# Turning r unscaled and multiplying the powers of the decay in where it leaves PSUM

## The reference

```
for t in range(768):
    cur   = (u * k[t]) outer v[t]
    y[t]  = r[t] @ (state + cur)
    state = w * state + k[t] outer v[t]
```

## Time and profile before

| | us |
|---|---|
| median of 3 runs | 996.05 (994.66 to 996.93) |
| profiled execution, first to last instruction (span) | 962.4 |
| median of the runs less that span | 33.65 |
| PE busy, of the span | 905.8 |
| POOL busy, of the span | 341.3 |
| DVE busy, of the span | 416.5 |
| ACT busy, of the span | 255.9 |

### The profile page before, as it was taken

One profiled execution on the slowest core, in us unless ns is written; L12 is line 12 of the kernel. 1 busy time (PEld: TensorE's weight loads), 2 busy tenths in 40 slices (PEclk: granted clock), 3 DMA queues, 4 the chain that ended last, 5 costly groups with the idle time before them and its releaser, 6 DMA issues.

```text
span 962.4 us, 19802 instructions
## 1 busy us (share of the span) xinstructions
PE 905.8 (94%) x6919; PEld 856.9 (89%) x6920; DVE 416.5 (43%) x697; ACT 255.9 (27%) x511; POOL 341.3 (35%) x276
## 2 busy tenths in 40 slices
PE   6899998898998999999979999999999999999998
PEld 6777787697897888988878999999999999999998
DVE  7767766536655547264244222222232223222221
ACT  1333332122222222222233222222222222222222
POOL 6799996577444326065346010010100001000000
PEclk9999999999999999999999999999999999999999
DMA  8885565353324132224221010000100001000000
GB/s 198 224 223 129 129 163 186 85 167 113 133 85 155 39 133 82 82 62 150 93 80 29 22 42 9 25 25 0 49 0 25 25 18 31 0 25 0 25 1 25
DMA packets 115583, 74.20 MB, mean 77 GB/s; under 512 B 79248, under 2 KB 109840, under 8 KB 115552
## 3 DMA queue, kind: packets, MB, share of 16 engines
q1 hardware_dynamic: 101312, 48.01, 18.2%
q10 hardware_dynamic: 10720, 14.95, 4.3%
q0 software_dynamic: 3520, 10.82, 4.0%
HBM read 57.44 MB, written 16.32 MB: 77 GB/s over the span
## 4 chain that ended last, share of the span: by engine, by line
PE 67%; POOL 12%; issue 7%; DVE 6%; DMA 3%; POOLq 2%; DVEq 1%; SPq 1%; ACT 1%; ACTq 0%
PE bank L1187 20%; PE bank L1189 20%; PE bank L1188 20%; POOL w_lo L501 3%; POOL w_lo L552 3%; DMA xs<-x_rows,token_of 2%; POOL k_pad L486 2%; POOL r_pad L488 2%; POOL ruk L491 2%; PE bank L1239 1%; PE bank L1083 1%; POOL xs L531 1%; POOLq L549 1%; SPq L401 1%; DVE w_hi L832 1%
## 5 line engine op out<-in xcount | busy, mean ns | idle before, releaser
L1187 PE MATMUL bank<-bT_hi,f_hi 128*128 (+1 forms) x576 | 194.7, 338 | 0.0
L1188 PE MATMUL bank<-bT_lo,f_hi 128*128 (+1 forms) x576 | 192.8, 335 | 0.0
L1189 PE MATMUL bank<-bT_hi,f_lo 128*128 (+1 forms) x576 | 192.6, 334 | 0.0
L890 DVE TENSOR_TENSOR act<-silu,bank 128x384 f32<-128x384 f32 x96 | 53.2, 554 | 252.1 <-PE bank L1189 252.1
L552 POOL TENSOR_TENSOR w_lo<-raw,w_hi x72 | 99.0, 1408 | 111.1 <-DVE w_hi L832 107.0
L571 POOL DMA_INDIRECT xg<-y_slots,slot_of x24 | 25.0, 1040 | 277.4 <-DVE xg_s L874 256.2
L1188 PEld LDWEIGHTS bank<-bT_lo,f_hi 128*128 128x128 f32 x576 | 108.5, 188 | 0.0
L1187 PEld LDWEIGHTS bank<-bT_hi,f_hi 128*128 128x128 f32 x576 | 108.4, 188 | 0.0
L1189 PEld LDWEIGHTS bank<-bT_hi,f_lo 128*128 128x128 f32 x576 | 108.4, 188 | 0.0
L1187 PE MATMUL bank<-f_hi,act_hi 128*128 128x384 f32 x288 | 96.8, 336 | 2.5 <-DVE act_lo L893 2.5
L1189 PE MATMUL bank<-f_hi,act_lo 128*128 128x384 f32 x288 | 96.7, 336 | 0.0
(11 more groups left out here) (169 smaller groups left out, 1464.6 us busy)
## 6 DMA issues: line engine op xcount, KB each, us to landing
raw<-in_moe_w_dram SPq DMA_DIRECT2D x16, 1536.0 KB, 6.7
y_slots<-y_out ACTq DMA_DIRECT2D x28, 192.0 KB, 1.9
k_in<-in_k_dram SPq DMA_DIRECT2D x24, 192.0 KB, 2.7
r_in<-in_r_dram SPq DMA_DIRECT2D x24, 192.0 KB, 3.5
v_in<-in_v_dram SPq DMA_DIRECT2D x24, 192.0 KB, 3.7
x_rows<-x_out ACTq DMA_DIRECT2D x24, 192.0 KB, 1.9
out_dram<-o_out ACTq DMA_DIRECT2D x7, 576.0 KB, 3.0
f_raw<-in_moe_w_gate_dram SPq DMA_DIRECT2D x12, 192.0 KB, 2.6
```

Of the source, the lines that this page charges most:

```text
L890: dve.tensor_tensor(act[:, par, :], silu[:, par, :], bank[2 * par + 1][:, 0:BN], ALU.mult).then_inc(act_made, 1)
L1187: pe.matmul(ps, a_hi, b_hi_, start=first, stop=False)
L1188: pe.matmul(ps, a_hi, b_lo_, start=False, stop=False)
L1189: return pe.matmul(ps, a_lo, b_hi_, start=False, stop=last)
```

## The change

r is loaded straight into a buffer that is padded to 64 channels a head (r_in becomes 128 x 4 x 8 x 64; the pads are zeroed once by DVE). POOL no longer makes r_pad; PE turns the raw r_in of the step. The instruction that takes the turned r out of PSUM moves from ACT (a copy) to DVE, where it is a multiplication by the powers z, which are laid out with channels in rows already. It is the new function r_out(i): it is called for step i+1 inside DVE's step i, between the masks and the sum of ruk. The powers are now laid out by pairs (4 columns of 128 rows, padded), so that z serves r_out directly, pow_r is gone, and w^128 is one squaring of w^64 from z. The padded w is now loaded first, by two DMAs.

```diff
 sp:
-            sp.dma_start(w_col[:], w.rearrange("h d -> (h d)")...).then_inc(w_in, 16)
+            sp.wait_ge(w_pad_clear, 1)
+            for i in range(2):
+                sp.dma_start(w_pad[i * HALF:i * HALF + D, :], w.rearrange("(q i) d -> i d q", i=2)[i], ...
...
+            sp.wait_ge(r_pads_clear, 1)
             load_qkv(0, 0)
 pool:
-                wait(pool, turned, 2 * (i - 1))
+                wait(pool, turned, 2 * (i - 1) - 1)
                 pool.tensor_tensor(k_pad[:, par, :, 0:D], heads(k_in[:, b, :]), pow_k[:, :, 0:D],
                                    ALU.mult).then_inc(scaled, 1)
-                pool.tensor_tensor(r_pad[:, par, :, 0:D], heads(r_in[:, b, :]), heads(pow_r[:]),
-                                   ALU.mult).then_inc(scaled, 1)
                 wait(pool, bonus_sum, i)
 dve:
-            dve.memset(w128[:], 0.0).then_inc(w_pad_clear, 1)
+            dve.memset(w_pad[:], 1.0).then_inc(w_pad_clear, 1)
+            dve.memset(r_in[:, :, :, D:HALF], 0.0).then_inc(r_pads_clear, 1)
...
-            while n < P:
-                dve.tensor_tensor(w128[:], w128[:], w128[:], ALU.mult).then_inc(setup_step, 1)
+            dve.tensor_tensor(w128[:], z[:, :, P:P + 1]..., z[:, :, P:P + 1]..., ALU.mult).then_inc(setup_step, 1)
...
+            def r_out(i):
+                dve.wait_ge(turned, 2 * i + 2)
+                dve.tensor_tensor(rT[:].rearrange("p (q t) -> p q t", q=PAIRS),
+                                  bank[1][:].rearrange("p (q t) -> p q t", q=PAIRS), z[:, :, 0:P],
+                                  ALU.mult).then_inc(rT_made, 1)
...
                     dve.copy_predicated(attn[:, half, :, :], ...).then_inc(masked, 1)
+                if not (at_end(c, CH - 1) and b == B - 1):
+                    r_out(i + 1)
                 dve.wait_ge(ruk_made, i + 1)
 act:
-                act_e.copy(kT[:], bank[0][:]).then_inc(turned_out, 1)
-                act_e.wait_ge(turned, 2 * i + 2)
-                act_e.copy(rT[:], bank[1][:]).then_inc(turned_out, 1)
+                act_e.copy(kT[:], bank[0][:]).then_inc(kT_made, 1)
 pe:
-                pe.wait_ge(scaled, 2 * i + 2)
-                wait(pe, turned_out, 2 * i)
+                pe.wait_ge(scaled, i + 1)
+                wait(pe, kT_made, i)
...
+                wait(pe, rT_made, i)
+                for q in range(PAIRS):
+                    mm = pe.transpose(bank[1][:, q * P:(q + 1) * P],
+                                      r_in[:, b, 2 * q:2 * q + 2, :].rearrange("p h d -> p (h d)"), ident[:])
+                mm.then_inc(turned, 1)
```

More of the change, by code:

```diff
@@ L166, in build @@
         w128 = here("w128", [P, PAIRS], F32)
+        w_pad = here("w_pad", [P, PAIRS], F32)
         zeros_at = cursor[0]
@@ L169, in build @@
         region(raw_at + 2 * slot_bytes)
-        r_in = here("r_in", [P, B, DM], F32)
+        r_in = here("r_in", [P, B, H, HALF], F32)
         k_in = here("k_in", [P, B, DM], F32)
         v_in = here("v_in", [P, B, DM], F32)
-        bonus_u = here("bonus_u", [P, DM], F32)
-        pow_r = here("pow_r", [P, DM], F32)
-        pow_k = here("pow_k", [P, DM], F32)
+        pow_k = here("pow_k", [P, H, HALF], F32)
         assert cursor[0] <= work_at
@@ L179, in build @@
         k_pad = here("k_pad", [P, 2, H, HALF], F32)
-        r_pad = here("r_pad", [P, 2, H, HALF], F32)
+        z = here("z", [P, PAIRS, P + 1], F32)
         state = here("state", [P, B, PAIRS, PW], F32)
@@ L185, in build @@
         ruk_sum = here("ruk_sum", [P, H], F32)
+        bonus_u = here("bonus_u", [P, DM], F32)
         region(work_at + 18 * 1024)
[L188 to L191, removed]
+        z_inv = here("z_inv", [P, PAIRS, P], F32)
+        w_inv = here("w_inv", [P, PAIRS], F32)
         region(work_at)
@@ L280, in build @@
         w_pad_clear = sem("w_pad_clear")
+        r_pads_clear = sem("r_pads_clear")
         w_pad_in = sem("w_pad_in")
@@ L292, in build @@
         turned = sem("turned")
-        turned_out = sem("turned_out")
+        kT_made = sem("kT_made")
+        rT_made = sem("rT_made")
         scored = sem("scored")
@@ L395, in _ @@
         def _(sp):
-            sp.dma_start(w_col[:], w.rearrange("h d -> (h d)").rearrange("(c p) -> p c", p=P),
-                         allow_slow_non_contiguous=True).then_inc(w_in, 16)
+            sp.wait_ge(w_pad_clear, 1)
+            for i in range(2):
+                sp.dma_start(w_pad[i * HALF:i * HALF + D, :], w.rearrange("(q i) d -> i d q", i=2)[i],
+                             allow_slow_non_contiguous=True).then_inc(w_pad_in, 16)
             def load_qkv(c, b):
-                for src, dst in ((k, k_in), (r, r_in), (v, v_in)):
-                    sp.dma_start(heads(dst[:, b, :]),
+                for src, dst in ((k, heads(k_in[:, b, :])), (r, r_in[:, b, :, 0:D]), (v, heads(v_in[:, b, :]))):
+                    sp.dma_start(dst,
                                  src[b].rearrange("h t d -> t h d")[bass.ds(c * P, P)]).then_inc(loaded[b], 16)
+            sp.wait_ge(r_pads_clear, 1)
             load_qkv(0, 0)
@@ L409, in _ @@
                          allow_slow_non_contiguous=True).then_inc(router_in, 16)
[L411 to L414, removed]
             def load_w1(e, half, landed):
@@ L475, in _ @@
             pool.memset(k_pad[:], 0.0).then_inc(pads_clear, 1)
-            pool.memset(r_pad[:], 0.0).then_inc(pads_clear, 1)
-            pool.wait_ge(pads_clear, 2)
+            pool.wait_ge(pads_clear, 1)
             def attention_step(c, b):
@@ L484, in attention_step @@
                 wait(pool, state_mm, min(i - 1, STATES) if isinstance(i, int) else i - 1)
-                wait(pool, turned, 2 * (i - 1))
-                pool.tensor_tensor(k_pad[:, par, :, 0:D], heads(k_in[:, b, :]), heads(pow_k[:]),
-                                   ALU.mult).then_inc(scaled, 1)
-                pool.tensor_tensor(r_pad[:, par, :, 0:D], heads(r_in[:, b, :]), heads(pow_r[:]),
+                wait(pool, turned, 2 * (i - 1) - 1)
+                pool.tensor_tensor(k_pad[:, par, :, 0:D], heads(k_in[:, b, :]), pow_k[:, :, 0:D],
                                    ALU.mult).then_inc(scaled, 1)
                 wait(pool, bonus_sum, i)
-                pool.tensor_tensor(ruk[:], r_in[:, b, :], bonus_u[:], ALU.mult).then_inc(ru_made, 1)
+                pool.tensor_tensor(heads(ruk[:]), r_in[:, b, :, 0:D], heads(bonus_u[:]), ALU.mult).then_inc(ru_made, 1)
                 pool.wait_ge(ru_made, i + 1)
@@ L505, in flat @@
                 return t[:].rearrange("p a b -> p (a b)")
-            pool.wait_ge(pow_copied, 2)
+            pool.wait_ge(pow_copied, 1)
             pool.wait_ge(u_in, 16)
@@ L607, in _ @@
             step = 2
-            dve.wait_ge(w_in, 16)
-            dve.tensor_copy(z[:, :, HALF + 1:HALF + 2], w_col[:].unsqueeze(2)).then_inc(setup_step, 1)
+            dve.wait_ge(w_pad_in, 32)
+            dve.tensor_copy(z[:, :, HALF + 1:HALF + 2], w_pad[:].unsqueeze(2)).then_inc(setup_step, 1)
             step += 1
@@ L614, in _ @@
                 dve.tensor_tensor(z[:, :, HALF + m + 1:HALF + 2 * m + 1], z[:, :, HALF + 1:HALF + m + 1],
-                                  z[:, :, HALF + m:HALF + m + 1].to_broadcast([P, KC, m]),
+                                  z[:, :, HALF + m:HALF + m + 1].to_broadcast([P, PAIRS, m]),
                                   ALU.mult).then_inc(setup_step, 1)
@@ L622, in _ @@
             dve.wait_ge(setup_step, step)
-            dve.tensor_tensor(z[:, :, 0:HALF], z[:, :, HALF:P], w_inv[:].unsqueeze(2).to_broadcast([P, KC, HALF]),
+            dve.tensor_tensor(z[:, :, 0:HALF], z[:, :, HALF:P], w_inv[:].unsqueeze(2).to_broadcast([P, PAIRS, HALF]),
                               ALU.mult).then_inc(z_ready, 1)
@@ L628, in _ @@
             dve.wait_ge(z_turned, 1)
-            dve.tensor_copy(pow_r[:], bank[0][:, 0:DM]).then_inc(pow_copied, 1)
-            dve.wait_ge(z_turned, 2)
-            dve.tensor_copy(pow_k[:], bank[1][:, 0:DM]).then_inc(pow_copied, 1)
+            dve.tensor_copy(pow_k[:].rearrange("p h d -> p (h d)"), bank[1][:]).then_inc(pow_copied, 1)
             dve.memset(attn[:], 0.0).then_inc(clears_made, 1)
@@ L636, in _ @@
             dve.wait_ge(clears_made, 6)
-            dve.wait_ge(w_pad_in, 32)
-            n = 1
-            while n < P:
-                dve.tensor_tensor(w128[:], w128[:], w128[:], ALU.mult).then_inc(setup_step, 1)
-                step += 1
-                dve.wait_ge(setup_step, step)
-                n *= 2
+            dve.tensor_tensor(w128[:], z[:, :, P:P + 1].rearrange("p q o -> p (q o)"),
+                              z[:, :, P:P + 1].rearrange("p q o -> p (q o)"), ALU.mult).then_inc(setup_step, 1)
+            step += 1
+            dve.wait_ge(setup_step, step)
             for i in range(2):
@@ L682, in attention_step @@
                 dve.tensor_tensor(x_out[:, b, :], bank[4][:, 0:DM], cv[:], ALU.add).then_inc(x_made, 1)
+            r_out(0)
             for c in rounds(dve, 0, CH - 1):
```

(29 more changed lines are left out.)

1 line of the change is left out of this document (removed).

## The result

The change makes the kernel slower. In the comparison that the prediction was made for, the changed kernel took 1016.38 us (median of 4 runs, 1011.68 to 1019.66) and the kernel before 995.36 (4 runs), a ratio of 1.0221, 95% interval 1.0182 to 1.026, or +21.0 us. On a later occasion the same two took 989.13 (5 runs) and 966.8 (17 runs): 1.0247, interval 1.022 to 1.0273, +22.3 us. The forecast was 1021 and +25.3.

What follows compares the result with a forecast made beforehand. Before, POOL (5.71 us a step) and PE (5.54) bound the attention; after, a one-step ring of 7.30 us. Its 19 periods give +23.2, the start +2.1, total +25.3 on 996.05: 1021 us, eight in ten from 1011 to 1034.

Steps and rivals of the forecast that it cites:

- The ring: Attention, ruk_sum(i) to ruk_sum(i+1) through POOL, PE and r_out on DVE: closes within one step, not two, 7.30 us.
- The period: Attention, from one ruk on POOL to the next: 7.30 us against 6.08 before, 19 times, +23.2 us.
- The bounds: Attention step: 7.11 or 6.73 us with faster POOL products, 7.62 us with w_lo at 1.55.
- the prediction's signs: Middle of attention: POOL waits 2 us for ruk_sum, PE idles 1.8, period 7.3, clock 1.00, w_lo 1.27, r_out 0.68.
- The start: Up to ruk of step 4: loading w, the powers and the first chunk's steps add 2.1 us, bounds 0 and +3.7.
- The term for w: Start of the kernel: two DMAs taking 2.6 us land w at 4.0 instead of 3.02, +1.0 us.
- the term of before: Attention of the kernel before, ruk(4) to ruk(23): 115.54 us for 19 periods, 6.08 us each.
- these stalls: Attention of the kernel before: some small DMA stalls, included in its 6.08 us a period, given no size of their own.
- The level: Whole kernel: median of runs 33.65 us above the span, so 987.7 of span becomes 1021.3 us.
- The clock: Rival: PE's clock falls in the gap ahead of each turn, 0.85 us each, 16 us on top, 1037; chance 0.14.
- DVE's chain: Rival: in attention, x_out, r times state, turn, r_out and sum bind at 5.86 us a step, about 994; chance 0.05.

Runs made afterwards that it cites:

- With r_pad in the ring: Kernel before, with the turned r copied out of PSUM by DVE ahead of the sum of ruk, POOL still making r_pad: 1016.64 us.
- with w_lo out of it: Changed kernel, with POOL's piece of w_lo moved ahead of its wait for the sum: 966.59 us, 1.0008 of the kernel before.
- opened by r_out's place: Changed kernel, with r_out(i+1) moved behind the sum of ruk and cv on DVE: 959.55 us, 0.9937 of the kernel before.
- closed over two steps: Changed kernel, with two buffers for ruk and r_out still ahead of the sum: 960.42 us, 0.9944 of the kernel before.
- the later profile: Changed kernel, unchanged, timed and profiled again against the kernel before: 989.13 us, ratio 1.0247, span 985.0.

## Why the prediction was right

*The ring* was the prediction's main step, and every edit that opened, shortened or lengthened it moved the period as its terms say. With r_pad in the ring it was 8.2 undisturbed (8.3 expected), with w_lo out of it 6.03 to 6.12 (6.1), opened by r_out's place 5.72 undisturbed (5.5 to 5.8), closed over two steps 6.03 (5.7 to 6.1). The first chunk has no w_lo, and its last three periods in the later profile are 6.04 to 6.05 (6.07 in the prediction).

*The period* was forecast at 7.30 and measured 7.32 and 7.25. r_out took 0.69 (0.68), the turn 1.09, the sum 0.54. The bounds were put as if the terms were free of each other. They are not: in one step of four ruk ran at 1.00, cv was held to 1.36, the state's decay started late, and w_lo took 1.58 beside it; in the other three ruk took 1.38, cv 0.56 and w_lo 1.27. In those three the terms came one by one as forecast. In the fourth, which is the turn printed above, two are off, ruk by -0.38 and w_lo by +0.32, and nearly cancel. So 29 of the 38 periods of the two profiles were 7.19 to 7.26, and none was under 7.04. Of the prediction's signs two were missed by little: the granted clock was 0.98 and 0.97 and not 1.00, and PE idled 1.03 us ahead of the turn for k_pad and not 1.8, with 0.35 more a step ahead of r times the state, for x_out. The rule of the Trainium skill (SBUF — State Buffer, "Who interferes with whom") agrees with these rows: the DVE instructions that go together with a longer one on POOL are cv and the state's decay, with two inputs in SBUF, and r_out, with one in PSUM, kept its 0.69 throughout.

*The start* was put at +2.1, bounds 0 and +3.7. ruk of step 4 came 3.28 us later than before in one pair of profiles and 0.57 in the other. The term for w was too large: the two DMAs took 1.9 us to land, not 2.6, and DVE started at 3.36 us, +0.34 against 3.02, not +1.0. The difference between the two profiles of the changed kernel goes with PE's clock, which the prediction counted in one turn only: in the first profile the scores of steps 0 and 2 took 2.08 us, where 1.16 is usual, and the granted clock from 20 to 40 us was 0.83; in the later one they took 1.16 and it was 1.00.

*What was off by 3 to 4 us* (+25.3 forecast, +21.0 and +22.3 measured) is in the main the term of before: 6.08 a period, from one profile that had hardly a stall (0.3 us), where the later one has 6.35. That first profile, 962.4 us and 1.8 around it, is an execution of 964.2, and the median of before is 966.8 on the later occasion: 2.6 of the 3.0 us there. The kernel before runs into the loads of the experts' weights in some executions and then into PE's lower clock; in the changed kernel, slower, v had landed in time in both profiles. The prediction called these stalls small and did not count that the change would hide them. That they set the mean difference is argued from two profiles of before and from how its runs go with the clock, not shown run by run. For the first occasion (+21.0) there is no profile of before to read.

*The level* was right for a wrong reason. The prediction took the 33.65 us between span and runs as time around the span, to be added. It is 1.8 us. The rest was a difference between occasions, and it did no harm: the median of before that the difference was added to comes from the same occasion as the result. On the later occasion the same +25.3 would have given 992.1, against 989.13.

*The rivals.* The clock does fall in the gap of the ring, but rarely, and costs at most 2 us there and not 16. DVE's chain at 5.86 exists: its waits are the ones left with two buffers for ruk, at 6.03. It needed the buffer that the change doesn't have. Taking r_pad off POOL is worth something, as the change intends, once the ring is open.

## What to carry to other kernels

When an instruction that waits is put into an in-order queue, list what stands behind it and who waits for that, and follow it until it comes back: then count in how many steps the ring closes. A wait that costs nothing over two steps can cost the whole surplus over one. The cure is a place behind whatever others wait for, or one more buffer, and either turned +22 us into -6 here, both into -11. A short wait can also cost more than itself: where PE sat idle 2.87 and 3.17 us behind a late load, it ran at the lower clock for 9.6 us after it.

## What the runs showed that was not expected

The same kernel before ran 29 us apart on two occasions (995 and 966 us). The later occasions were on three chips (965.89, 966.8 and 966.55 us), the chip of the first is not on record. The one profile of the slow occasion, the changed kernel's, shows PE, ACT and DVE almost at a standstill for some 20 us while POOL issues its indirect DMAs:

```profile
238.57 0.48 PE L1185 MATMUL bank<-w_hi,hT_hi 128*128 x1 [1.64 <-issue]
240.68 0.48 PE L1186 MATMUL bank<-w_lo,hT_hi 128*128 x1 [1.64 <-issue]
243.47 0.48 PE L1187 MATMUL bank<-w_hi,hT_lo 128*128 x1 [2.30 <-issue]
```

The granted clock there is 0.62 in the mean, and no engine is named as releaser of these matmuls, only "issue". POOL's DMAs by themselves are not it: in the stretch of the later profile POOL is busy 17.3 us with them as well, and PE is busy all of the 28 us. What held the engines is open. The kernel before has no profile of 995 us, so that it lost its 29 us in the same place is likely and not shown.
